# Weighing V in fp16 pairs inside clustered attention

## The chip, the cores and the metric

One core of one Trainium2 chip runs the whole program. The metric is device time in microseconds, of the slowest core where there are several; here there is one.

## What is computed

Clustered attention, followed by two layers of experts (top-1 routing of 1536 tokens). Only attention is touched by the change:

```python
scores = scale * np.matmul(q, k.transpose(0, 1, 3, 2))      # q, k, v: 2 x 8 x 768 x 64, fp32
scores = np.where(q_assign == k_assign, scores, -1e9)       # cluster = argmax over 16 centroids
attn = np.exp(scores - scores.max(-1))
attn = attn / (attn.sum(-1) + 1e-9)
out = np.matmul(attn, v)
```

A query none of whose keys is in its cluster gets the mean of V. The result is fp32.

## The kernel before

The program has a raw program for each engine, with semaphores between them; nothing is moved by a scheduler, so every engine does its work in the order in which it is written. `attention` goes over 16 heads (2 batches of 8) one after the other. `steps` (L163) calls `step(s, par)` for s = -1, 0, 1, then a rolled loop for heads 2 to 13, then 14 and 15. Step s holds three heads at once: the scores and the weighing of head s, the cluster masks and the row maxima of head s + 1, and the turning and cluster logits of head s + 2. `has(s, n)` says whether head s + n exists. `par` chooses one of two buffers.

A head has 768 keys in T = 6 tiles of 128 (`kt`), and 768 queries in two halves of 384 (`HALF`).

- TensorE, `step` (L516): `scores` (L481) makes the transposed scores of a tile of keys in two parts, an exact fp32r part with hi and lo of q and k (`QA`, `KA`) and one with `QB`, `KB`, whose rows hold the hi halves, the masks and the negated row maxima in three parts. `weigh` (L496) multiplies the exps of one key tile (`probs`, fp32, weights of 128 columns) with V and a column of ones (`v1`, 65 columns) and adds into the PSUM tile `pv`, three products for each half. Between these, `other` pops work of the next heads from the list `between`: `turn_b` (L455, transposed masks), twelve products of `maxima` (L463, u = 0 to 11, which alternate between the PSUM tiles `turn0` and `turn1`), four `turn_a` (L431), `turn_m` (L473, transposed maxima). How many go where is the table `BETWEEN` (L154). At the end of a step stands `assign` (L441), the cluster logits.
- ScalarE: the exps of a tile (L245, two of 384), behind tile 1 the masks into `QB` (L250), behind tile 2 `hi` (L225 and L226), at the end the two copies of `QA` (L232) and the maxima into `QB` (L258).
- VectorE: masks into `KB` (L376), twelve reductions of the maxima (L382), seven small operations that each wait for the one before (L388 to L395), two copies of `KA` (L349), the denominators and the output of the head (L403 to L410), the masks of head s + 2 (L356 to L364), the sum of V (L343).
- GpSimd: `lo` (L273 and L274: q and k less their hi halves), `double_hi` (L282 and L285: copies to other partitions), the sum of two output parts (L306), the copy of V into `v1` (L293).
- SyncE: q, k and v of head s + 2 (L199), behind the last head the first experts' weights (L1133) and the copies of x.

An exp may start when its buffer of `probs` (two) is free and the scores are there; `scores` of tile kt waits for the exps of tile kt - 2; `weigh` waits for the exps of its half. `turn_m` waits for the seven small operations, `assign` for the copies of `QA` and `KA`.

## Time and profile before

| | us |
|---|---|
| runs, median of 3 (lowest to highest) | 748.81 (747.76 to 752.83) |
| the profiled execution | 747.8 |
| its span | 746.1 |

| engine | busy us | share of the span | instructions |
|---|---|---|---|
| TensorE, products (PE) | 724.5 | 97% | 5200 |
| TensorE, weight loads (PEld) | 643.3 | 86% | 5209 |
| VectorE (DVE) | 443.8 | 59% | 917 |
| ScalarE (ACT) | 247.2 | 33% | 441 |
| GpSimd (POOL) | 172.1 | 23% | 229 |

The span is counted from the first instruction to the last; the profiled execution is 1.7 us longer than it. Weight loads overlap products, and products overlap each other, so the time between two starts on TensorE, not the duration of one, tells what a product costs. Attention ends at about 326 us, and the rest are the two layers of experts. A row of a timeline gives start, length, engine, line, operation, `out<-in` and, in square brackets, how long the engine was idle before it and what it waited for.

### The profile page before, as it was taken

The numbers are of one execution on the slowest core, as the hardware profiler recorded it, in microseconds if no ns is written. First come the engines' busy times: TensorE is split into PE (matmuls) and PEld (weight loads), VectorE is DVE, ScalarE is ACT, GpSimd is POOL, SyncE is SP. The second block draws the span as 40 slices with busy tenths as digits, with TensorE's granted clock in tenths as the row PEclk, the third lists the DMA queues.
The fourth block names the chain that finished last, engine by engine and source line by source line (L and its number), as shares of the span: only waits on it lengthen the run. The fifth ranks groups of instructions, "written<-read, shape, count | busy, mean of one in ns | idle before, by whom it ended". The sixth has DMA issues, their size and how long they took to land.

```text
span 746.1 us, 15191 instructions
## 1 busy us (share of the span) xinstructions
PE 724.5 (97%) x5200; PEld 643.3 (86%) x5209; DVE 443.8 (59%) x917; ACT 247.2 (33%) x441; POOL 172.1 (23%) x229
## 2 busy tenths in 40 slices
PE   8999999999999999997999999988999999999996
PEld 4799999999999999974898989945799998999995
DVE  5788888888888888546644655527533442624521
ACT  2344444444444444442214351313221232321300
POOL 4222222222222222001221312200222221312211
PEclk9999999999999999999999999999999999999998
DMA  3001110111011197041656998455445646662100
GB/s 99 18 18 33 32 33 31 32 32 32 32 32 32 32 341 309 1 165 34 232 185 233 365 325 313 145 203 204 143 156 167 231 170 233 256 231 92 40 28 29
DMA packets 43598, 99.16 MB, mean 133 GB/s; under 512 B 5139, under 2 KB 11283, under 8 KB 43568
## 3 DMA queue, kind: packets, MB, share of 16 engines
q1 hardware_dynamic: 36096, 84.45, 31.8%
q0 software_dynamic: 4544, 12.70, 5.4%
q10 hardware_dynamic: 2928, 1.62, 0.7%
q8 instruction: 17, 0.28, 0.2%
q14 instruction: 13, 0.11, 0.0%
HBM read 87.64 MB, written 13.11 MB: 135 GB/s over the span
## 4 chain that ended last, share of the span: by engine, by line
PE 49%; DVE 3%; DMA 2%; issue 1%; ACT 0%; POOL 0%; POOLq 0%; ACTq 0%; DVEq 0%
PE hT_ps_layer L1009 25%; PE y_ps_layer L1022 6%; PE y_ps_layer L1026 6%; PE y_ps_layer L1029 6%; PE x_turn_layer L996 2%; DMA x<-x_mid 1%; PE hT_ps_layer L951 1%; PE hT_ps_layer L938 1%; PE hT_ps_layer L936 1%; PE x_turn_layer L926 1%; DVE row_one_hot_layer L838 0%; DMA x_tile_layer<-x_src,token_to_read_layer 0%; DMA x_mid<-y_out_layer,y_token_layer 0%; PE count_ps_layer L926 0%; PE rank_ps_layer L926 0%
## 5 line engine op out<-in xcount | busy, mean ns | idle before, releaser
L1009 PEld LDWEIGHTS hT_ps_layer<-xT_layer,w 128*128 128x128 f32 x1664 | 189.6, 192 | 3.4 <-DVE xT_layer L871 1.4
L1009 PE MATMUL hT_ps_layer<-xT_layer,w 128*128 128x128 f32 x1664 | 190.2, 276 | 0.5 <-issue 0.5
L505 PE MATMUL pv<-v_and_one,probs 128*128 128x65 f32 x1152 | 147.9, 270 | 0.0
L505 PEld LDWEIGHTS pv<-v_and_one,probs 128*128 128x128 f32 x1152 | 146.8, 192 | 0.6
L382 DVE TENSOR_REDUCE max_halves<-turn 128x1 f32<-128x384 f32 x192 | 102.4, 555 | 39.3 <-PE turn L470 35.6
L245 ACT ACTIVATE probs<-scores 128x384 f32<-128x384 f32 x192 | 82.0, 492 | 85.2 <-PE scores L491 84.8
L760 ACT ACTIVATE hT_hi_layer<-hT_ps_layer 128x512 fp32r<-128x512 f32 x52 | 31.1, 597 | 238.9 <-PE hT_ps_layer L1009 238.9
L898 DVE SCALAR_TENSOR_TENSOR hT_lo_layer<-hT_ps_layer,hT_hi_layer 128x512 fp32r<-128x512 f32 x52 | 34.7, 689 | 88.0 <-ACT hT_hi_layer L760 75.5
L878 DVE TENSOR_TENSOR w_lo<-w,w_hi 128x1024 fp32r<-128x1024 f32 x64 | 74.0, 1220 | 0.0
L755 ACT ACTIVATE w_hi<-w 128x1024 fp32r<-128x1024 f32 x64 | 62.4, 1047 | 27.0 <-issue 27.0
L470 PE MATMUL turn<-kB,qB 96*128 96x384 f32 x192 | 69.8, 402 | 0.0
L1022 PE MATMUL y_ps_layer<-w_hi,hT_hi_layer 128*128 128x512 f32 x208 | 58.6, 404 | 0.0
L1029 PE MATMUL y_ps_layer<-w_hi,hT_lo_layer 128*128 128x512 f32 x208 | 56.6, 394 | 0.0
L1026 PE MATMUL y_ps_layer<-w_lo,hT_hi_layer 128*128 128x512 f32 x208 | 56.5, 394 | 0.0
L1073 POOL DMA_INDIRECT out_dram<-y_out_layer,y_token_layer x16 | 19.8, 1239 | 148.1 <-DVE y_out_layer L909 148.1
L909 DVE TENSOR_SCALAR y_out_layer<-y_ps_layer,slot_gate_layer 128x512 f32<-128x512 f32 x16 | 12.0, 751 | 64.1 <-PE y_ps_layer L1029 64.1
L491 PE MATMUL scores<-qA,kA 128*128 128x384 f32 x192 | 49.7, 353 | 0.0
L491 PE MATMUL scores<-qB,kB 99*128 99x384 f32 x192 | 47.0, 340 | 0.0
L1026 PEld LDWEIGHTS y_ps_layer<-w_lo,hT_hi_layer 128*128 128x128 f32 x208 | 39.1, 188 | 9.0
L1029 PEld LDWEIGHTS y_ps_layer<-w_hi,hT_lo_layer 128*128 128x128 f32 x208 | 38.9, 188 | 9.1 <-DVE hT_lo_layer L898 0.5
L1022 PEld LDWEIGHTS y_ps_layer<-w_hi,hT_hi_layer 128*128 128x128 f32 x208 | 37.2, 189 | 6.7
L282 POOL CAST qB<-qA 64x768 fp32r<-64x768 f32 x16 | 13.1, 817 | 125.4 <-DVE kA L349 125.4
(194 smaller groups left out, 864.7 us busy)
## 6 DMA issues: line engine op xcount, KB each, us to landing
w<-in_moe_w_dram SPq DMA_DIRECT2D x32, 2048.0 KB, 9.6
qkv_raw<-in_q_dram SPq DMA_DIRECT2D x16, 192.0 KB, 2.4
qkv_raw<-in_k_dram SPq DMA_DIRECT2D x16, 192.0 KB, 2.5
qkv_raw<-in_v_dram SPq DMA_DIRECT2D x16, 192.0 KB, 3.2
x_src<-x SPq DMA_DIRECT2D x2, 1536.0 KB, 11.9
x_mid<-x SPq DMA_DIRECT2D x2, 1536.0 KB, 14.7
...
```

The lines of the kernel that those rows point to most:

```text
L245: nc.scalar.activation(probs[kt % 2][:, n * HALF:(n + 1) * HALF], sc[kt % 2][:, n, 0:HALF], ACT.Exp, scale=SCALE).then_inc(probs_ready, 1)
L382: nc.vector.tensor_reduce(mh[:, u // 2, u % 2:u % 2 + 1], turn[b][:, 0:HALF], AX.X, ALU.max).then_inc(turn_free[b], 1)
L470: nc.tensor.matmul(turn[b][:, 0:HALF], QB[par][0:ROWS_MASK, t * P:(t + 1) * P], KB[par][0:ROWS_MASK, n * HALF:(n + 1) * HALF], start=True, ...
L491: m = nc.tensor.matmul(sc[kt % 2][:, n, 0:HALF], lhs[:, kt * P:(kt + 1) * P], rhs[:, n * HALF:(n + 1) * HALF], start=(part == 0), stop=(pa ...
L505: m = nc.tensor.matmul(pv_o[:, t, :], probs[kt % 2][:, t * P:(t + 1) * P], v1[par][:, kt, :], start=False, stop=(kt == T - 1), skip_group_ ...
L755: nc.scalar.activation(W2H[par][:, c, :], W2[par][:, c, :], ACT.Copy).then_inc(w2_hi, 1)
L878: nc.vector.tensor_tensor(W2L[:, c, :], W2[par][:, c, :], W2H[par][:, c, :].bitcast(F32), ALU.subtract).then_inc(w2_lo, 1)
L898: nc.vector.scalar_tensor_tensor(out=hL[:, half, :].rearrange("p c n -> p (c n)"), in0=hp[n][:], scalar=0.0, in1=hH[:, half, :].rearrange( ...
L1009: t = nc.tensor.matmul(hp[n][:, i * P:(i + 1) * P], W1[par][:, c, f * P:(f + 1) * P], xT[:, c, :], start=(c == 0), stop=(c == CD - 1))
L1022: nc.tensor.matmul(yp[:], hH[:, f, :], W2H[par][:, f, :], start=(f == 0), stop=False)
L1026: nc.tensor.matmul(yp[:], hH[:, f, :], W2L[:, f, :], start=False, stop=False)
L1029: t = nc.tensor.matmul(yp[:], hL[:, f, :], W2H[par][:, f, :], start=False, stop=(f == CF - 1))
```

## The change

The exps of a tile are made twice from the same scores, once in fp32 (`probs`) and once in fp16 (`p_hi`). The rest `probs - p_hi` is taken in fp16 (`p_lo`) by GpSimd for tiles 0 to 4 and by VectorE for tile 5. V is scaled by a power of two and split into `v_hi` (ScalarE) and `v_lo` (VectorE), both fp16. In place of one fp32 product stand three of 16 bit: `p_hi` with `v_hi`, `p_hi` with `v_lo`, `p_lo` with `v_hi`. The first two of a half are `weigh_hi`, the third is `weigh_lo`, which stands one tile later. `probs`, `p_hi` and `p_lo` have three buffers. The sum of V is made on TensorE by twelve products with ones (`sum_v`), not by VectorE.

All of V is loaded at the start by ScalarE's queue in four quarters into the memory of the experts' W1 (`v_all`). VectorE takes the largest absolute value of each quarter (`v_topmost`), then of all (`v_power`, with one transposition on TensorE, `turn_v`), and makes from its exponent bits the factors `v_up` and `v_down`. The exponents are raised by 7 with the maxima (`SHIFT`).

Moved: the copies of `KA` from VectorE to ScalarE (`evac_a`, now four); `double_hi` from GpSimd to two DMAs of SyncE; the factor of the masks from VectorE to ScalarE's copy; the load of the first two W1 behind the last `v_lo`; GpSimd's sum of a head's output into the next step; `BETWEEN` has five places for each tile.

```diff
-    BETWEEN = ((0, 0, 1), (0, 1, 1), (1, 2, 1), (1, 2, 1), (2, 2, 0), (2, 1, 0))
+    BETWEEN = ((0, 0, 0, 0, 0), (0, 0, 0, 1, 0), (0, 0, 0, 1, 1), (1, 0, 1, 1, 1), (1, 1, 1, 1, 0), (1, 1, 1, 0, 0))
...
+            def double_hi(i, par):
+
+                b, m = use_a(i, 3)
+                sp.wait_ge(turn_free[b], m + 1)
+                sp.dma_start(QB[par][0:D, :].bitcast(F32), QA[par][0:D, :].bitcast(F32)).then_inc(hi_doubled, 16)
+                sp.dma_start(KB[par][0:D, :].bitcast(F32), KA[par][D:2 * D, :].bitcast(F32)).then_inc(hi_doubled, 16)
...
+            def split_v(i, par):
+                act.wait_ge(v_scaled, 1)
+                wait(act, pv_done, T * (i - 1))
+                nc.scalar.activation(v_hi[par][:, :, 0:D], v_of(i), ACT.Copy, scale=v_up).then_inc(v_hi_done, 1)
...
                         for n in range(2):
+                            half = slice(n * HALF, (n + 1) * HALF)
                             act.wait_ge(scored[kt % 2], T * s + 2 * (kt // 2) + n + 1)
-                            nc.scalar.activation(probs[kt % 2][:, n * HALF:(n + 1) * HALF], sc[kt % 2][:, n, 0:HALF],
-                                                 ACT.Exp, scale=SCALE).then_inc(probs_ready, 1)
+                            nc.scalar.activation(probs[slot][:, half], sc[kt % 2][:, n, 0:HALF], ACT.Exp, scale=SCALE).then_inc(probs_ready, 1)
+                            nc.scalar.activation(p_hi[slot][:, half], sc[kt % 2][:, n, 0:HALF], ACT.Exp, scale=SCALE).then_inc(probs_ready, 1)
...
+                    if kt == 3 and has(s, 1) and not first:
+                        split_v(s + 1, 1 - par)
...
+                if first:
+                    split_v(0, 0)
             run(act, step)
...
+            def rest(i, kt):
+
+                slot = kt % RING_P
+                wait(pool, pv_done, T * i + kt - RING_P + 1)
+                for n in range(2):
+                    half = slice(n * HALF, (n + 1) * HALF)
+                    pool.wait_ge(probs_ready, 4 * (T * i + kt) + 2 * n + 2)
+                    nc.gpsimd.tensor_tensor(p_lo[slot][:, half], probs[slot][:, half], p_hi[slot][:, half], ALU.subtract).then_inc(p_lo_pool, 1)
...
+                if c:
+                    rest(s, 0)
+                    rest(s, 1)
+                if c and not (isinstance(s, int) and s == 0):
+                    add_up(s - 1)
+                if c:
+                    rest(s, 2)
+                if a:
+                    lo_q(s + 2, par)
+                if c:
+                    rest(s, 3)
+                if a:
+                    lo_k(s + 2, par)
+                if c:
+                    rest(s, 4)
...
-                link(nc.vector.tensor_tensor(eq[:], lg[:], top[:, 1, :].unsqueeze(2).to_broadcast([P, 2 * T, C]), ALU.is_equal))
-                if par is not None:
-                    nc.vector.tensor_scalar(maskb[par][:, :, 0:C], eq[:, 0:T, :], MASKED, None, ALU.mult).then_inc(mask_steps, 1)
-                    nc.vector.tensor_scalar(maskb[par][:, :, 2 * C:3 * C], eq[:, T:2 * T, :], -1.0, 1.0, ALU.mult, ALU.add).then_inc(mask_steps, 1)
...
+                best = lambda n: top[:, 1, n:n + T].unsqueeze(2).to_broadcast([P, T, C])
+                nc.vector.tensor_tensor(maskb[par][:, :, 0:C], lg[:, 0:T, :], best(0), ALU.is_equal).then_inc(mask_steps, 1)
+                nc.vector.tensor_tensor(maskb[par][:, :, 2 * C:3 * C], lg[:, T:2 * T, :], best(T), ALU.not_equal).then_inc(mask_steps, 1)
...
+                        if u == 5 and first:
+                            v_topmost(2)
+                        if u == 9 and not first:
+                            split_v(i, 1 - par)
...
+                if first:
+                    v_topmost(3)
+                    v_power()
+                    split_v(0, 0)
                 if has(s, 0):
+                    kt = T - 1
+                    slot = kt % RING_P
+                    dve.wait_ge(pv_done, T * s + kt - RING_P + 1)
+                    for n in range(2):
+                        half = slice(n * HALF, (n + 1) * HALF)
+                        dve.wait_ge(probs_ready, 4 * (T * s + kt) + 2 * n + 2)
+                        nc.vector.tensor_tensor(p_lo[slot][:, half], probs[slot][:, half], p_hi[slot][:, half], ALU.subtract).then_inc(p_lo_dve, 1)
                     dve.wait_ge(pv_done, T * s + T)
...
+            def weigh_hi(i, par, kt, half):
+                pe.wait_ge(probs_ready, 4 * (T * i + kt) + 2 * half + 2)
                 for t in range(half * T // 2, (half + 1) * T // 2):
-                    m = nc.tensor.matmul(pv_o[:, t, :], probs[kt % 2][:, t * P:(t + 1) * P], v1[par][:, kt, :],
+                    p = p_hi[kt % RING_P][:, t * P:(t + 1) * P]
+                    nc.tensor.matmul(pv_o[:, t, :], p, v_hi[par][:, kt, 0:D + 1], start=False, stop=False, skip_group_check=True)
+                    m = nc.tensor.matmul(pv_o[:, t, 0:D], p, v_lo[par][:, kt, :], start=False, stop=False, skip_group_check=True)
...
+            def weigh_lo(i, par, kt, half):
+                if kt == T - 1:
+                    pe.wait_ge(p_lo_dve, 2 * i + half + 1)
+                else:
+                    pe.wait_ge(p_lo_pool, POOL_P * i + 2 * kt + half + 1)
+                for t in range(half * T // 2, (half + 1) * T // 2):
+                    m = nc.tensor.matmul(pv_o[:, t, :], p_lo[kt % RING_P][:, t * P:(t + 1) * P], v_hi[par][:, kt, 0:D + 1],
                                          start=False, stop=(kt == T - 1), skip_group_check=True)
...
                 for kt in range(T):
...
+                    for half in range(2):
+                        if c and kt > 0:
+                            weigh_lo(s, par, kt - 1, half)
+                        other(BETWEEN[kt][2 * half])
+                        if c:
+                            weigh_hi(s, par, kt, half)
+                        if half == 0:
+                            other(BETWEEN[kt][1])
+                    other(BETWEEN[kt][3])
                     if c and kt + 2 < T:
                         scores(s, par, kt + 2, last)
-                    other(BETWEEN[kt][2])
+                    other(BETWEEN[kt][4])
                 other(len(between))
+                if c:
+                    for half in range(2):
+                        weigh_lo(s, par, T - 1, half)
                 if a:
                     assign(s + 2, par)
+                if first:
+                    turn_v()
```

How this moves instructions is shown at three places. The line numbers of the rows after the change are those of the changed kernel.

ScalarE, the exps of tiles 1 and 2 of a head (`probs` and `probs_hi`) with the masks' copy `qB` between them. Before:

```order
L245 ACTIVATE probs<-scores 128x384 x4
L250 ACTIVATE qB<-turn 32x768
L245 ACTIVATE probs<-scores 128x384 x2
L225 ACTIVATE q_features<-qkv_raw 128x6x64
L226 ACTIVATE k_features<-qkv_raw 128x6x64
```

ScalarE at the same place after the change; the first four rows are tile 1, tile 0 has four more like them ahead:

```order
L304 ACTIVATE probs<-scores 128x384
L305 ACTIVATE probs_hi<-scores 128x384
L304 ACTIVATE probs<-scores 128x384
L305 ACTIVATE probs_hi<-scores 128x384
L309 ACTIVATE qB<-turn 32x768
L304 ACTIVATE probs<-scores 128x384
L305 ACTIVATE probs_hi<-scores 128x384
L304 ACTIVATE probs<-scores 128x384
L305 ACTIVATE probs_hi<-scores 128x384
L273 ACTIVATE q_features<-qk_raw 128x6x64
```

Ahead of the masks' copy stand eight exps where four stood, and ahead of the copy of q twelve where six stood.

TensorE around the first products of the maxima (`turn<-kB,qB`), from the transposed masks on. Before:

```order
L460 MATMUL turn<-ident_b,masks 96x128 x6
L505 MATMUL pv<-v_and_one,probs 128x65 x6
L470 MATMUL turn<-kB,qB 128x384
L491 MATMUL scores<-qA,kA 128x384 x2
L491 MATMUL scores<-qB,kB 128x384 x2
```

TensorE there after the change, up to the first product of the maxima; the last rows before it are `weigh_hi` of tile 2:

```order
L555 MATMUL turn<-ident_b,masks 96x128 x6
L586 MATMUL scores<-qA,kA 128x384 x2
L586 MATMUL scores<-qB,kB 128x384 x2
L615 MATMUL pv<-v_hi_and_one,probs_lo 128x65 x3
...
L605 MATMUL pv<-v_lo,probs_hi 128x64
L565 MATMUL turn<-kB,qB 128x384
L586 MATMUL scores<-qA,kA 128x384 x2
```

The first product of the maxima moved from behind the products of tile 1 to behind those of tile 2.

VectorE at the end of a head, from the small operations of the maxima to the denominator. Before:

```order
L394 CAST max_parts<-max_rest 128x6
L395 TENSOR_TENSOR max_parts<-max_rest,max_parts 128x6
L349 CAST kA<-turn 128x384 x2
L403 SCALAR_TENSOR_TENSOR denominator<-pv,no_key 128x6
L405 RECIPROCAL denominator<-denominator 128x6
```

VectorE there after the change:

```order
L481 CAST max_parts<-max_rest 128x6
L482 TENSOR_TENSOR max_parts<-max_rest,max_parts 128x6
L494 TENSOR_TENSOR probs_lo<-probs,probs_hi 128x384 x2
L498 SCALAR_TENSOR_TENSOR denominator<-pv,no_key 128x6
L500 RECIPROCAL denominator<-denominator 128x6
```

In the place of two copies that TensorE's `assign` waits for stand two subtractions that its last `weigh_lo` of the head waits for.

## Rows read from the trace of the kernel before

**Rows 1.** The page, part 1: busy us, share of the span, instructions.
```profile
PE 724.5 (97%) x5200; PEld 643.3 (86%) x5209; DVE 443.8 (59%) x917; ACT 247.2 (33%) x441; POOL 172.1 (23%) x229
```

**Rows 2.** Timeline of TensorE in one step: start us, us, engine, line, operation, tiles.
```profile
150.40 0.78 PE L505 MATMUL pv<-v_and_one,probs 128*128 128x65 f32 x6
150.98 0.42 PE L470 MATMUL turn<-kB,qB 96*128 96x384 f32 x1
...
161.04 0.84 PE L451 MATMUL cluster_logits_ps<-centroids_T,qA 128*128 x6
...
162.40 0.94 PE L491 MATMUL scores<-qA,kA 128*128 128x384 f32 x4
...
166.35 0.53 PE L460 MATMUL turn<-ident_b,masks 128*96 128x128 bf16 x6
166.72 1.50 PE L505 MATMUL pv<-v_and_one,probs 128*128 128x65 f32 x12
...
181.11 0.94 PE L491 MATMUL scores<-qA,kA 128*128 128x384 f32 x4
```

**Rows 3.** Timeline of TensorE in the routing of the first experts.
```profile
351.44 0.56 PE L986 MATMUL rank_ps_layer<-tile_gate_parts_layer,row_one_hot_layer 128*128 128x72 bf16 x12 [0.86 <-DVE tile_gate_parts_layer L859]
351.84 1.46 PE L951 MATMUL hT_ps_layer<-blank 128*128 128x512 bf16 x6
```

**Rows 4.** Timeline of ScalarE in the same step as rows 2.
```profile
148.96 0.87 ACT L245 ACTIVATE probs<-scores 128x384 f32<-128x384 f32 x2
149.72 0.53 ACT L225 ACTIVATE q_features<-qkv_raw 128x384 fp32r<-128x384 f32 x1
...
163.55 1.64 ACT L245 ACTIVATE probs<-scores 128x384 f32<-128x384 f32 x4 [1.67 <-PE scores L491]
166.92 0.80 ACT L250 ACTIVATE qB<-turn 32x768 fp32r<-32x768 bf16 x1 [1.73 <-PE turn L460]
```

**Rows 5.** Timeline of VectorE in the same step.
```profile
151.44 0.56 DVE L382 TENSOR_REDUCE max_halves<-turn 128x1 f32<-128x384 f32 x1 [0.29 <-PE turn L470]
152.29 1.69 DVE L382 TENSOR_REDUCE max_halves<-turn 128x1 f32<-128x384 f32 x3 [0.29 <-PE turn L470]
...
158.24 0.17 DVE L388 TENSOR_REDUCE max_negated<-max_halves 128x6 f32<-128x12 f32 x1
...
159.79 1.02 DVE L349 CAST kA<-turn 128x384 fp32r<-128x384 f32 x2
160.73 0.15 DVE L403 SCALAR_TENSOR_TENSOR denominator<-pv,no_key 128x6 f32<-128x6 f32 x1
...
163.96 0.54 DVE L358 TENSOR_TENSOR cluster_best<-cluster_logits,cluster_top 128x192 f32<-128x192 f32 x1
...
166.14 0.81 DVE L343 TENSOR_REDUCE v_sum<-qkv_raw 128x64 f32<-128x384 f32 x1
```

**Rows 6.** Timeline of GpSimd in the same step.
```profile
163.26 1.03 POOL L306 TENSOR_TENSOR x<-o_attn,o_mean 128x384 f32 x1 [0.48 <-DVE o_mean L410]
164.23 0.64 POOL L293 COPY v_and_one<-qkv_raw 128x384 f32<-128x384 f32 x1
```

**Rows 7.** Durations of two lines of VectorE: ns min/median/max, first and last start.
```profile
L358 DVE TENSOR_TENSOR cluster_best<-cluster_logits,cluster_top x16: 357/542/549, 14.5 to 295.2; 128x192 f32<-128x192 f32 x16
...
L406 DVE TENSOR_SCALAR denominator<-no_key x16: 171/670/686, 48.6 to 323.7; 128x6 f32<-128x6 f32 x16
```

**Rows 8.** Timeline before the first head: VectorE, then ScalarE.
```profile
27.43 0.17 DVE L395 TENSOR_TENSOR max_parts<-max_rest,max_parts 128x6 bf16<-128x6 f32 x1
...
30.82 1.28 ACT L245 ACT_TABLE_LOAD   x1
32.42 1.64 ACT L245 ACTIVATE probs<-scores 128x384 f32<-128x384 f32 x4 [0.32 <-PE scores L491]
```

**Rows 9.** The page, part 6: DMA issues, count, KB each, us to landing.
```profile
w<-in_moe_w_dram SPq DMA_DIRECT2D x32, 2048.0 KB, 9.6
qkv_raw<-in_q_dram SPq DMA_DIRECT2D x16, 192.0 KB, 2.4
```

234 lines of the change are left out of this document (137 added, 97 removed).

## The prediction

> **What bounds the kernel now.** First the page's busy times, then the timeline of one step of one head engine by engine, then the durations by line. The page says that TensorE is busy 97% of the span [rows 1]. TensorE's timeline shows why: a step begins with `scores` at 162.40 and the next one at 181.11, so a step is 18.7 us, and inside it no matmul row carries an idle time [rows 2]. The other engines wait for TensorE: ScalarE's rows before an exp or before `L250` end in `<-PE scores`, `<-PE turn` [rows 4], VectorE's reductions have 0.29 us of `<-PE turn` ahead of it [rows 5], and of GpSimd's operations, six a step, [rows 6] show the last two. So the step is TensorE's sum, and 15 such steps (heads 0 to 14) stand between the start and the last head. Behind attention nothing is changed except when the first experts' weights come.
>
> **TensorE's part.** Three fp32 products of one half take 150.98 - 150.40 = 0.58 us [rows 2]; a step has 12 halves, 7.0 us, which go. In their place stand 108 products with 16 bit operands and 12 for `sum_v`, 120 in all, each with a 128 column weight load. The trace has no 65 column fp16 product. The nearest row is twelve bf16 products of 72 columns with 128 column weights, all inputs ready: the next line starts 351.84 - 351.44 = 0.40 us later, 0.033 each [rows 3]. The other end is `L460`, six with 96 column weights and 128 moving columns in 166.72 - 166.35 = 0.37, 0.062 each [rows 2]. I take 0.033: 120 x 0.033 = 4.0 us, and TensorE's sum falls to 18.7 - 7.0 + 4.0 = 15.7 us. With 0.062 it is 19.1.
> The Trainium skill, "TensorE: Matmul & The Clock Gate", section "Back-to-back issue gap", speaks against this: it gives about 81 ns per product for a stream of weight load and product at 128 columns. By that page 120 products would be 9.7 us and TensorE's sum 21.4. The row at 72 columns measures 33 ns, so the row decides.
>
> **What takes TensorE's place.** TensorE's sum would allow 15.7 us, but the step is a ring of waits, and the change lengthens the other engines' part of it. I walk it, t = 0 at the start of `scores`.
> 1. The first exp starts at 163.55 - 162.40 = 1.15 [rows 2, 4]. Exps follow each other in 0.38 us (two in 149.72 - 148.96 = 0.76) [rows 4]. Each tile is now exponentiated twice, so tiles 0 and 1 are eight exps, not four: the last starts at 1.15 + 7 x 0.38 = 3.8 and is done at 4.3 (0.49 for one).
> 2. `turn_b` stands behind `weigh_hi(1, half 1)` on TensorE, which needs that last exp: six products, 0.2 us, so it starts at 4.6. `L250` starts 166.92 - 166.35 = 0.57 after `turn_b` [rows 2, 4], at 5.2, and takes 0.80. The exps of tile 2 are queued behind it on ScalarE: 6.0 to 6.0 + 3 x 0.38 + 0.49 = 7.6.
> 3. The first of the 12 maxima products stands behind `weigh_hi(2, half 1)`, which needs them: t = 7.9. Before, it stood right behind the products of tile 1, ahead of everything that waits for tile 2.
> 4. VectorE's reduction starts 151.44 - 150.98 = 0.46 after its product [rows 2, 5], at 8.4. Three in a row take 1.69, so 0.565 each [rows 5], twelve 6.8 us. `split_v` stands behind the tenth, two gaps, 0.5 together, come from the `scores` that stand between maxima products: 8.4 + 6.8 + 0.55 + 0.5 = 16.2.
> 5. The seven small operations take 159.79 - 158.24 = 1.55 [rows 5]: t = 17.8. `turn_m` waits for them, as before.
> 6. New: VectorE then subtracts the rests of tile 5, two operations, and `weigh_lo(5)` waits for them. Their form is not in the trace; 192 elements of this kind take 0.357 [rows 7], a reduction of 384 takes 0.56 [rows 5]. I take 0.55 each: 18.9. The two `kA` copies that stood here (1.02) [rows 5] are gone, but those were hidden under TensorE's products; what replaces them is waited for.
> 7. `weigh_lo(5)` takes 0.1, and `assign` behind it 162.40 - 161.04 = 1.36 [rows 2]. The next `scores` start at 18.9 + 0.1 + 1.36 = 20.4.
> So the step is 20.4 us instead of 18.7: plus 1.7, times 15 = 25.5 us.
>
> **What is hidden.** ScalarE's sum per step is 24 exps x 0.38 = 9.1, six copies of 384 at no more than 0.53 = 3.2 [rows 4], `L250` and `L258` 1.6, `split_v` 0.5: 14.4 of 20.4. The tail of a head on VectorE, from `L403` to the masks' end, is 166.14 - 160.73 = 5.4 [rows 5], less one operation of the form of `L358` (0.357 alone [rows 7]) that goes. It starts 0.2 behind `weigh_lo(5)`, at t = -1.1, and ends at 4.0, when `turn_b` at 4.6 has not yet come: hidden by 0.6 us, and lost one for one behind that. `v_sum` (0.81) goes, it was hidden. The doubling of q and k by SyncE's DMA instead of GpSimd starts at t = 18.5 and is needed at 7.9 of the next step, 9.8 us later, and 192 KB land in 2.4 [rows 9]; queued behind it on SyncE are only the loads of the next q and k. W1 now waits for the last `v_lo`, in the step before the last: it is needed behind the routing, so I count nothing.
> GpSimd gets ten subtractions per step. Two operations of 384 elements start 164.23 - 163.26 = 0.97 apart [rows 6]; bounds 0.6 (the copy lasts 0.64) and 1.03. With 0.97 its order is ten rests, two of q and k, one sum: the first at t = 2.1, the twelfth (tile 4, half 0) done at 2.1 + 12 x 0.97 = 13.7, and with what VectorE takes from it 14.5. TensorE needs it for the eleventh maxima product at about 14.7: just in time. At 1.03 it is 15.3, and 0.3 us on the step.
>
> **Start and end.** Before the first head VectorE takes the top of V in four reductions of 1536 elements, each 0.56 + 1152 elements at the pace of 384 in 0.4, 1.75 us. Two of them lie in waits. The third stands in the maxima, the fourth behind the small operations, whose last one ends at 27.6 [rows 8]: 27.6 + 3.5 = 31.1. Then 2 small operations, a transposition, a reduction and 8 small operations, 0.2 each with 0.7 for the passes over TensorE: 34.0. ScalarE's `split_v` stands ahead of the exps and of their table load: 34.0 + 0.5 + 1.28 = 35.8 for the first exp, 32.42 before [rows 8]. That is 3.4 us. A quarter of V is 768 KB, and 2048 KB land in 9.6 [rows 9], so V's load beside the first q and k adds between 0 and 3.6; I take 0.5, since q's and k's own 192 KB are issued at the same time. The last head has no other work to mix in: 24 exps and 11 GpSimd operations end at about its old length, I take plus 0.5.
> Sum: 25.5 + 3.9 + 0.5 = 29.9 us. The profiled execution took 747.8 us (span 746.1); 747.8 + 29.9 = 777.7. The median of the runs is 1.0 above it, 748.8: so 779 us.
>
> **The rivals.**
> A, faster: the ring has more slack than I see, and the step follows TensorE. TensorE's 15.7 and the wait at the step's end, from its last transposition to the rests of tile 5, about 1.5: 17.2 us. 15 x (17.2 - 18.7) = -22.5, and 4.4 for start and end: 748.8 - 18 = 731 us. For it speaks that the trace's rings have waits everywhere on the other engines (VectorE is busy 59%). Against it: steps 1 to 3 above have no free choice, they are queue orders. It decides if the first maxima product comes before t = 6. Chance 0.11.
> B, the same ring a little shorter, the rest of the step 18.5 to 19.2: within 1%. Chance 0.07.
> C, slower still: GpSimd and VectorE get in each other's way. `L406`, six elements, takes 171 ns at the least and 670 in the median; `L358` 357 and 542 [rows 7]; the `L358` of 0.54 at 163.96 [rows 5] lies on GpSimd's two operations from 163.26 to 164.87 [rows 6]. Now GpSimd works 13 x 0.97 = 12.6 us of a step, not some 5, and beside it stand on VectorE four mask operations, `split_v` and, if GpSimd is late, the small operations. If each of the two sides waits for the other, GpSimd's twelfth operation is done at 15.4, the eleventh maximum starts 0.7 later, and three small operations wait 0.1 to 0.5 each: 21.4 us. 15 x 2.7 + 4.4 = 45: 793 us. Chance 0.13.
> The Trainium skill, "SBUF — State Buffer", section "Who interferes with whom", says that a VectorE instruction with two inputs in SBUF, or in a two-port mode, and a GpSimd instruction that reads SBUF block each other for the whole instruction. The 670 against 171 ns agree. It is the mechanism of C.
> D, the change doesn't do what it says: three 16 bit products cost TensorE as much as one of fp32, because each has its own weight load. At 0.062 us each (`L460`) TensorE's sum is 19.1, above the old 18.7, and the seven groups of products that stand on the ring grow by 0.5: a step of 20.9, 15 x 2.2 + 4.4 = 37, 786 us. Against it stands [rows 3]. Chance 0.05. By the 81 ns of the page named above the sum alone would be 21.4, which would make it some 794 us.
>
> **How the numbers follow.** The forecast 0.64, A 0.11, B 0.07, C 0.13, D 0.05. The forecast's own range: maxima product 0.5 earlier or later, rests 0.36 to 0.9, GpSimd 0.6 to 1.03, the start 0 to 8: 19.6 to 21.0 us a step, 764 to 790 us. To leave out no more than 2 in 10 the range reaches down to 756, towards B (741 to 756 stay outside), and up over C's own 793 to 796. A measurement of this kernel tells about 1% from no change. Faster by over 1%: A, 0.11. Within 1%: 0.07. Slower: 0.82.
>
> **What would show it.** In the profile after: the distance between two starts of `scores` at a head's begin (20.4); the first `L470` product of a step near t = 7.9, with TensorE idle before it on ScalarE's exps; `weigh_lo(5)` waiting for VectorE's rests; twelve fp16 products in 0.4 us; the first exp at 35.8. Wrong if TensorE is still without idle time in a step (A or D), or if GpSimd's rests end TensorE's waits at tile 2 to 4 (C).

## The result, and the profile after

| | kernel before | kernel after |
|---|---|---|
| median of the runs | 749.09 us (747.76 to 752.83) | 779.77 us (777.82 to 782.19) |
| ratio, 95% interval | | 1.040 (1.036 to 1.045) |
| profiled execution: own time, span | 747.8, 746.1 us | 782.2, 780.5 us |
| mean granted clock of TensorE over the span | 0.992 (1.00 in every step of attention) | 0.973 |

The kernel is 4.0% slower. Medians are over all runs and ratios over the undisturbed ones: of the experiments below, those of 814.5 and 754.4 us have one run in a slower state in their median. The profiled execution was 2.4 us above the median, so what follows adds up to 34.4 us and not to 30.7. First the page's busy times of after, which answer to [rows 1]:

```profile
PE 713.3 (91%) x5937; PEld 587.2 (75%) x5946; DVE 447.1 (57%) x916; ACT 342.0 (44%) x681; POOL 277.7 (36%) x341
```

TensorE's busy time fell by only 11 us. That is not the work taken out: a row's length reaches past the start of the next one, so short gaps count as busy, and a step at a lower clock counts longer. What changed is that TensorE is no longer busy throughout, 91% where it was 97%. The timeline of TensorE in one step of after (columns as in [rows 2]):

```profile
162.65 0.96 PE L586 MATMUL scores<-qA,kA 128*128 128x384 f32 x4
...
167.24 0.53 PE L555 MATMUL turn<-ident_b,masks 128*96 128x128 bf16 x6
...
169.56 0.20 PE L604 MATMUL pv<-v_hi_and_one,probs_hi 128*128 128x65 f16 x1 [0.92 <-ACT probs_hi L305]
...
170.33 0.20 PE L604 MATMUL pv<-v_hi_and_one,probs_hi 128*128 128x65 f16 x1 [0.32 <-ACT probs_hi L305]
170.37 0.20 PE L605 MATMUL pv<-v_lo,probs_hi 128*128 128x64 f16 x1
...
170.63 0.41 PE L565 MATMUL turn<-kB,qB 96*128 96x384 f32 x1
...
181.03 0.50 PE L615 MATMUL pv<-v_hi_and_one,probs_lo 128*128 128x65 f16 x6
181.55 0.84 PE L546 MATMUL cluster_logits_ps<-centroids_T,qA 128*128 x6
...
182.91 0.96 PE L586 MATMUL scores<-qA,kA 128*128 128x384 f32 x4
```

The step is 182.91 - 162.65 = 20.26 us. A 16 bit product starts 0.04 after its neighbour (170.33, 170.37). Before the first maxima product `L565` TensorE now waits for ScalarE's second exps, which [rows 2] did not show. ScalarE and VectorE in the same step:

```profile
163.82 0.49 ACT L304 ACTIVATE probs<-scores 128x384 f32<-128x384 f32 x1 [2.13 <-PE scores L586]
...
166.43 0.56 ACT L305 ACTIVATE probs_hi<-scores 128x384 f16<-128x384 f32 x1
167.81 0.80 ACT L309 ACTIVATE qB<-turn 32x768 fp32r<-32x768 bf16 x1 [0.82 <-PE turn L555]
168.64 0.49 ACT L304 ACTIVATE probs<-scores 128x384 f32<-128x384 f32 x1
...
178.83 1.03 ACT L280 ACTIVATE qA<-turn 128x384 fp32r<-128x384 f32 x2 [2.67 <-PE turn L533]
```

```profile
165.73 0.97 DVE L446 TENSOR_TENSOR masks<-cluster_logits,cluster_top 128x96 bf16<-128x96 f32 x1
...
171.08 0.56 DVE L465 TENSOR_REDUCE max_halves<-turn 128x1 f32<-128x384 f32 x1 [2.32 <-PE turn L565]
...
177.58 1.01 DVE L465 TENSOR_REDUCE max_halves<-turn 128x1 f32<-128x384 f32 x2
178.71 0.17 DVE L475 TENSOR_REDUCE max_negated<-max_halves 128x6 f32<-128x12 f32 x1
...
180.18 1.03 DVE L494 TENSOR_TENSOR probs_lo<-probs,probs_hi 128x384 f16<-128x384 f32 x2
```

Before, VectorE waited 0.56 us for the first maxima product of a step (the row below is from the step at 162.40) and 0.29 for later ones [rows 5]; now it waits 2.32 for the first.

```profile
168.49 0.56 DVE L382 TENSOR_REDUCE max_halves<-turn 128x1 f32<-128x384 f32 x1 [0.56 <-PE turn L470]
```

GpSimd in the step of after:

```profile
164.77 3.59 POOL L349 TENSOR_TENSOR probs_lo<-probs,probs_hi 128x384 f16<-128x384 f32 x4 [8.14 <-ACT probs_hi L305]
...
175.01 1.79 POOL L349 TENSOR_TENSOR probs_lo<-probs,probs_hi 128x384 f16<-128x384 f32 x2
```

Where the 34.4 us of the two profiled executions come from: the first exp starts 6.84 us later (39.26 against 32.42 [rows 8]); from there to the first operation behind head 14 (`L498`, before `L403`) it is 306.1 us against 277.1, plus 29.0; the last head takes 13.55 against 13.71; the rest 421.6 against 422.9. Most steps are 20.2 us, plus 1.5 each. Five are longer. The busy table by step, two ordinary ones and two of the five (the last three columns: granted clock, DMA share, GB/s):

```profile
141.14:161.31 20.17, 17.63 (x193) 13.83 (x193) 14.86 (x36) 14.24 (x34) 11.75 (x13) 1.00 0.14 39
161.31:181.57 20.26, 17.70 (x193) 13.86 (x193) 14.86 (x36) 14.28 (x34) 11.76 (x13) 1.00 0.13 39
181.57:202.62 21.05, 18.68 (x193) 14.97 (x193) 14.86 (x35) 14.10 (x34) 11.75 (x13) 0.92 0.13 37
98.63:120.89 22.26, 20.20 (x193) 16.46 (x193) 13.98 (x36) 14.00 (x34) 11.72 (x13) 0.85 0.13 37
```

VectorE, ScalarE and GpSimd are not busy longer in the two long steps; TensorE's clock is lower there and its busy time longer. The timeline shows where it falls, here at the end of the third:

```profile
198.45 0.82 PE L533 MATMUL turn<-ident,q_features 128*128 128x128 f32 x3 [0.54 <-DVE max_halves L465]
199.41 0.88 PE L533 MATMUL turn<-ident,q_features 128*128 128x128 f32 x3
200.09 1.69 PE L533 MATMUL turn<-ident,k_features 128*128 128x128 f32 x6
```

Behind a wait for the last maxima the six transpositions of k take 1.69 us, where they take 1.09 at full clock. One such wait does not decide it: the next step has the same one and keeps its clock.

```profile
219.50 0.52 PE L533 MATMUL turn<-ident,q_features 128*128 128x128 f32 x3 [0.54 <-DVE max_halves L465]
```

The five longer steps hold 5.3 us over the ordinary ones, and only four of them, with 4.5 us, are at a lower clock. The fifth (77.61 to 98.63, 21.02 us) has the granted clock at 1.00. There a VectorE operation of the masks that takes 0.36 alone stands beside GpSimd's rests, and TensorE waits for the masks:

```profile
80.86 1.11 DVE L442 TENSOR_TENSOR cluster_logits<-cluster_best,tie 128x192 f32<-128x192 f32 x1
```
```profile
83.90 0.53 PE L555 MATMUL turn<-ident_b,masks 128*96 128x128 bf16 x6 [0.41 <-DVE masks L446]
```

That is rival C's mechanism on the ring, in one step of fifteen.

### The profile page after: what moved, and what is told of

It is laid out like the page before. It is cut to its first block, busy times and chain, and to the rows that moved or that the text cites. A ratio compares the mean times of both kernels' runs of the same rounds, so it can differ in the third digit from the quotient of the medians.

```text
span 780.5 us, 17315 instructions
## 1 busy us (share of the span) xinstructions
PE 713.3 (91%) x5937; PEld 587.2 (75%) x5946; DVE 447.1 (57%) x916; ACT 342.0 (44%) x681; POOL 277.7 (36%) x341
## 3 DMA queue, kind: packets, MB, share of 16 engines
q10 hardware_dynamic: 5040, 4.77, 1.9%
## 4 chain that ended last, share of the span: by engine, by line
PE 47%; DVE 2%; DMA 2%; issue 1%; ACT 0%; POOL 0%; POOLq 0%; ACTq 0%; DVEq 0%
PE hT_ps_layer L1132 24%; PE y_ps_layer L1145 6%; PE y_ps_layer L1149 6%; PE y_ps_layer L1152 6%; PE x_turn_layer L1119 2%; DMA x<-x_mid 1%; PE hT_ps_layer L1074 1%; PE hT_ps_layer L1061 1%; PE hT_ps_layer L1059 1%; PE x_turn_layer L1049 1%; DVE row_one_hot_layer L961 0%; DMA x_tile_layer<-x_src,token_to_read_layer 0%; DMA x_mid<-y_out_layer,y_token_layer 0%; PE count_ps_layer L1049 0%; PE rank_ps_layer L1049 0%
## 5 line engine op out<-in xcount | busy, mean ns | idle before, releaser
L349 POOL TENSOR_TENSOR probs_lo<-probs,probs_hi 128x384 f16<-128x384 f32 x160 | 143.6, 922 | 151.6 <-ACT probs_hi L305 151.6
L465 DVE TENSOR_REDUCE max_halves<-turn 128x1 f32<-128x384 f32 x192 | 99.6, 553 | 48.0 <-PE turn L565 44.4
L304 ACT ACTIVATE probs<-scores 128x384 f32<-128x384 f32 x192 | 102.8, 535 | 33.0 <-PE scores L586 32.6
L305 ACT ACTIVATE probs_hi<-scores 128x384 f16<-128x384 f32 x192 | 104.5, 545 | 0.0
L604 PE MATMUL pv<-v_hi_and_one,probs_hi 128*128 128x65 f16 x576 | 63.0, 198 | 26.2 <-ACT probs_hi L305 25.3
L565 PE MATMUL turn<-kB,qB 96*128 96x384 f32 x192 | 79.1, 422 | 3.0 <-DVE max_halves L465 1.5
L604 PEld LDWEIGHTS pv<-v_hi_and_one,probs_hi 128*128 128x128 f16 x576 | 41.7, 99 | 42.0 <-ACT probs_hi L305 33.0
L1196 POOL DMA_INDIRECT out_dram<-y_out_layer,y_token_layer x16 | 19.7, 1233 | 147.1 <-DVE y_out_layer L1032 147.1
L605 PE MATMUL pv<-v_lo,probs_hi 128*128 128x64 f16 x576 | 61.6, 196 | 0.0
L586 PE MATMUL scores<-qA,kA 128*128 128x384 f32 x192 | 52.9, 372 | 0.0
L615 PE MATMUL pv<-v_hi_and_one,probs_lo 128*128 128x65 f16 x576 | 49.6, 197 | 2.8 <-POOL probs_lo L349 2.4
```

The source lines that it names most:

```text
L304: nc.scalar.activation(probs[slot][:, half], sc[kt % 2][:, n, 0:HALF], ACT.Exp, scale=SCALE).then_inc(probs_ready, 1)
L305: nc.scalar.activation(p_hi[slot][:, half], sc[kt % 2][:, n, 0:HALF], ACT.Exp, scale=SCALE).then_inc(probs_ready, 1)
L349: nc.gpsimd.tensor_tensor(p_lo[slot][:, half], probs[slot][:, half], p_hi[slot][:, half], ALU.subtract).then_inc(p_lo_pool, 1)
L465: nc.vector.tensor_reduce(mh[:, u // 2, u % 2:u % 2 + 1], turn[b][:, 0:HALF], AX.X, ALU.max).then_inc(turn_free[b], 1)
L565: nc.tensor.matmul(turn[b][:, 0:HALF], QB[par][0:ROWS_MASK, t * P:(t + 1) * P], KB[par][0:ROWS_MASK, n * HALF:(n + 1) * HALF], start=True, ...
L586: m = nc.tensor.matmul(sc[kt % 2][:, n, 0:HALF], lhs[:, kt * P:(kt + 1) * P], rhs[:, n * HALF:(n + 1) * HALF], start=(part == 0), stop=(pa ...
```

## The experiments

t is counted from the start of `scores` of a step. Ratios are to the kernel before, run beside each.

**Maxima products earlier.**
```diff
-BETWEEN = (..., (0, 0, 0, 1, 0), (0, 0, 0, 1, 1), (1, 0, 1, 1, 1), (1, 1, 1, 1, 0), (1, 1, 1, 0, 0))
+BETWEEN = (..., (0, 0, 0, 1, 2), (0, 0, 1, 1, 1), (1, 0, 1, 1, 1), (1, 1, 1, 0, 0), (1, 0, 0, 0, 0))
```


> The kernel after, with three maxima products placed ahead of the products of tile 2 that wait for ScalarE (two right behind scores(3), one between the halves of tile 2). Theory, the ring of waits: the first reduction moves from t = 8.43 to about 6.45 (L309 of the masks ends at 5.96, then product and 0.46), and everything behind it by the same 2.0 us: a step of 18.3 instead of 20.26, 15 x -1.95 = -29, so about 751 us. Rival C, GpSimd's ten rests set the step: it does not start its rests earlier, so 20.2 us a step and 780 us. Rival TensorE-bound: no change either, 780.

Measured: 757.4 us, ratio 1.014 (1.012 to 1.015), a step of 18.93 for the ordinary ones. That is 22 us by the medians, 20 by the ratios (1.040 to 1.014), of the change's 31, by the place of three products alone. The step is 0.6 us longer than expected, and the time 6 us. The rows of a step whose `scores` start at 152.71:

```profile
159.06 0.59 PE L565 MATMUL turn<-kB,qB 96*128 96x384 f32 x2 [0.47 <-DVE kB L459]
```
```profile
157.86 0.95 DVE L459 CAST kB<-turn 32x768 fp32r<-32x768 bf16 x1 [1.12 <-PE turn L555]
159.51 2.11 DVE L465 TENSOR_REDUCE max_halves<-turn 128x1 f32<-128x384 f32 x4 [0.69 <-PE turn L565]
...
165.30 1.09 DVE L431 SCALAR_TENSOR_TENSOR v_lo<-w,v_scale_bits,v_hi_and_one 128x384 f16<-128x384 f16 x1
```

The first reduction comes at 6.80, not 6.45: TensorE waits for VectorE's kB copy (0.95), which I had left out beside ScalarE's 0.80. And `split_v` takes 1.09 where it took 0.61: GpSimd's last two rests run from 165.05 to 167.16 here, beside it. The ring decides, and behind it contention is at work.

**The rests of tile 5 on GpSimd.**
```diff
+                    rest(s, 5)
...
-                        nc.vector.tensor_tensor(p_lo[slot][:, half], probs[slot][:, half], p_hi[slot][:, half], ALU.subtract)...
```


> The kernel after, with the rests of tile 5 on GpSimd instead of VectorE. Theory: VectorE's 1.03 us leave the ring, but ScalarE's four copies L280 end at t = 18.33 and assign waits for them, so the gain is cut to about 0.5 us: a step of 19.7, about 772 us. Rival C, GpSimd sets the step: two operations of 0.9 more on it make a step 1.8 longer, 22.0, about 806 us; in the weaker form, GpSimd and VectorE block each other on SBUF, the seven small operations behind the maxima (0.17 each, 1.43 together) now lie beside GpSimd's rests and grow to 0.5 each, and the step stays at 20.2 or above, 780 us or more.

Measured: 814.5 us, ratio 1.085 (1.080 to 1.089). The expectation of my theory was wrong by 42 us. The time is above the rival's 806 too. The rival's weaker form had the blocking, but on the seven small operations, which take 0.17 to 0.18 here; it falls on `split_v`. `split_v` over 14 steps (ns min/median/max), then TensorE and GpSimd in one of the steps of 24.5 us, and VectorE's row between them:

```profile
L429 DVE SCALAR_TENSOR_TENSOR v_lo<-w,v_scale_bits,v_hi_and_one x14: 606/1908/2062, 76.7 to 373.9; 128x384 f16<-128x384 f16 x12, 128x384 f16<-128x384 f32 x2
```
```profile
290.38 1.63 PE L577 MATMUL scores<-qA,kA 128*128 128x384 f32 x4
...
308.44 0.52 PE L524 MATMUL turn<-ident,q_features 128*128 128x128 f32 x3 [1.91 <-DVE max_halves L463]
...
309.74 1.69 PE L524 MATMUL turn<-ident,k_features 128*128 128x128 f32 x6
```
```profile
303.89 3.52 POOL L346 TENSOR_TENSOR probs_lo<-probs,probs_hi 128x384 f16<-128x384 f32 x4
```
```profile
305.85 1.98 DVE L429 SCALAR_TENSOR_TENSOR v_lo<-w,v_scale_bits,v_hi_and_one 128x384 f16<-128x384 f16 x1
```

GpSimd works on four rests without a pause from 303.89 to 307.41. VectorE's `split_v` starts within them and ends at 307.83, behind the last. TensorE waits 1.91 us for the maxima behind it, and then its clock falls: the six transpositions of k take 1.69 us and not 1.09. The step had also begun at the lower clock: its first four `scores` products, at 290.38, take 1.63 us and not 0.94. The one step with the clock at 1.00 throughout took 20.34 us, and in it `split_v` took 1.15; the others took 21.2 to 24.8 at clocks of 0.77 to 0.94. So the blocking (1.4 us in the step shown) and the lower clock together cost up to 4.5 us of a step.

**Both edits together.**

> Both edits together (maxima early, all rests on GpSimd). Theory: the last reduction ends at t = 14.0, the copies L280 at 16.5, assign right behind: a step of 17.9, 15 x -2.4 = -36, about 744 us, 4 to 5 us below the kernel before. If the two edits gave only the larger of their gains: 751. Rival C: as in the run with the rests alone, 780 or more, since GpSimd's twelve rests and three others are 13.5 us plus its waits and the last rest now starts behind all of them.

Measured: 770.4 us, ratio 1.031 (1.028 to 1.035), steps of 19.6. It lies between the theory's 744 to 751 and the rival's 780. GpSimd's rests start beside the masks, and the same blocking shows in other places:

```profile
158.32 1.12 DVE L440 TENSOR_TENSOR cluster_logits<-cluster_best,tie 128x192 f32<-128x192 f32 x1
...
172.18 0.84 DVE L475 TENSOR_SCALAR max_negated<-max_negated 128x6 f32<-128x6 f32 x1
```

Alone these take 0.36 and 0.17. `split_v` stands beside four rests here too, but takes 1.09 and not 1.98:

```profile
169.38 1.09 DVE L429 SCALAR_TENSOR_TENSOR v_lo<-w,v_scale_bits,v_hi_and_one 128x384 f16<-128x384 f16 x1
```
```profile
169.13 3.86 POOL L346 TENSOR_TENSOR probs_lo<-probs,probs_hi 128x384 f16<-128x384 f32 x4
```

The four rests take 3.86 where they took 3.52 in the run before: here VectorE waited for one of them and then GpSimd for VectorE, while there VectorE, starting in the third, waited for the third and the fourth. What decides between the two is open. The edits are not additive: moving the rests of tile 5 to GpSimd loses 13 us of the 20 that the earlier maxima win.

**One exp instead of two.**
```diff
-                            nc.scalar.activation(probs[slot][:, half], sc[kt % 2][:, n, 0:HALF], ACT.Exp, scale=SCALE)...
```


> The kernel after with ScalarE's twelve fp32 exps of a step left out: the fp32 probabilities are a constant 1.0, so the rests are 1 minus the high half; every rest, product and wait stays. Theory: tiles 0 and 1 are exponentiated by t = 2.8 instead of 4.34, but VectorE's masks end at 4.05 and set turn_b at 4.1 instead of 4.59; the copy L309 ends at 5.5, tile 2 has two exps and not four (6.4 instead of 7.62), and the first reduction starts at about 7.0 instead of 8.43: a step of 18.8, 15 x -1.4 = -21, about 759 us. Rival C, GpSimd's rests or their contention set the step: 20.2, 780 us.

Measured: 837.1 us, but this total can't be used: with other outputs of attention the experts got other tokens, and the page counts 1984 products of `hT` where after has 1664. Attention itself, to the same operation behind the last head, took 345.99 us against 358.90 in after. That is 12.9 less, not 21; the steps are 19.6 to 20.1, not 18.8. What cut the gain, in a step whose `scores` start at 156.43:

```profile
161.20 0.53 PE L558 MATMUL turn<-ident_b,masks 128*96 128x128 bf16 x6 [0.63 <-DVE masks L448]
```
```profile
158.31 0.98 DVE L444 TENSOR_TENSOR cluster_logits<-cluster_best,tie 128x192 f32<-128x192 f32 x1
...
160.10 0.96 DVE L448 TENSOR_TENSOR masks<-cluster_logits,cluster_top 128x96 bf16<-128x96 f32 x1
```

TensorE now waits for the masks, at t = 4.77: with the exps gone from there GpSimd starts its rests earlier (t = 1.73, where it was 2.12), and one more of VectorE's mask operations is blocked. My walk had the masks done at 4.05; they end at 4.63.

**Products of zeros in TensorE's waits.**
```diff
+            def keep_up(n):
+                for _ in range(n):
+                    nc.tensor.matmul(pv[:, 456:512], blank[:, 0:P], blank[:, 0:56], start=False, stop=False, ...)
```


> The kernel after, with products of zeros (56 columns, bf16, about 0.03 us each) in three of TensorE's waits in a step: 10 ahead of the high products of tile 1 (wait 0.41), 26 ahead of those of tile 2 (wait 0.92), 12 ahead of the first transposition of q behind the maxima (wait 0.54). They do nothing for the output. Theory that the idle gaps let TensorE's clock fall: the granted clock stays at full speed in all steps, the five steps of 21.0 to 22.3 become 20.2, and the time falls by 5 to 6 us, to about 774. Rival, the clock falls whatever TensorE does in these waits: 780 and again a mean clock of 0.97 to 0.98. If the products reach past the waits, up to 0.3 us a step, 4 us, come on top in either case.

Measured: 779.7 us, ratio 1.043 (1.042 to 1.044): no gain, by its number the rival's 780. In the profiled execution two steps are long (22.5 and 21.1) where after had five, but the rest took up to 20.35 and the mean clock was 0.975. It neither proves nor refutes the cause. The two runs with fp16 below do that for the kernel before; that the falls in after have the same cause is argued from them, not shown.

**TensorE's relief alone.**
```diff
-    v1 = [sb(f"v_and_one{i}", [P, T, D + 1], F32) for i in range(2)]
-    probs = [sb(f"probs{i}", [P, S], F32) for i in range(2)]
+    v1 = [sb(f"v_and_one{i}", [P, T, D + 2], F16) for i in range(2)]
+    probs = [sb(f"probs{i}", [P, S], F16) for i in range(2)]
```


> The kernel before, with probabilities, values and ones in fp16 and one product each: the rests are left out, and so is everything the change added to ScalarE, GpSimd and VectorE; the order is that of before. It shows what TensorE's relief alone is worth. Theory: TensorE's sum is 18.7 - 7.0 + 36 x 0.033 = 12.9, so the ring of the other engines decides: exps of tiles 0 and 1 done at 2.8, VectorE's masks at 3.8, turn_b, L250 from 4.4 to 5.2, the first reduction at 5.7 and the last end at 13.0, small operations 14.6, copies of k 15.7, assign 17.0. A step of 17.0, 15 x -1.7 = -26, about 722 us. Rival D, 16 bit products cost TensorE as much as the fp32 one (or 0.062 each): 18.7 a step or at most 1 us less, 733 to 747. If VectorE's and TensorE's order had the slack of rival A: 15 us a step, 693.

Measured: 754.4 us, ratio 1.008 (1.005 to 1.011). With 5.8 us of TensorE's work taken out of every step and nothing added the kernel is slightly slower than before, and 32 us above the expected 722. Two of its steps, busy times by engine:

```profile
89.00:106.64 17.64, 14.57 (x114) 11.29 (x112) 15.13 (x37) 8.42 (x18) 5.21 (x6) 1.00 0.11 34
124.50:145.70 21.20, 19.30 (x114) 15.41 (x112) 15.67 (x37) 8.42 (x18) 5.20 (x6) 0.69 0.09 28
```

At full clock a step is 17.7 us, and TensorE's waits in it are all for VectorE: 0.83 us for the masks, 0.92 for the `KB` copy, 0.42 for the `KA` copies, and three shorter ones for the reductions. So the ring through VectorE (15.1 us busy) stood 1.1 us behind TensorE's sum in the kernel before, and no relief of TensorE could bring more than that a step in this order. At the lower clock a step is 21.2.

**The same with products of zeros in its waits.**

> The kernel before with one fp16 product (rests left out, as in the run of that name), and with products of zeros (56 columns, bf16, about 0.03 us each) where TensorE waited there: 20 ahead of turn_b (wait 0.81), 26 ahead of the first maxima product (0.92), 14 ahead of the last products of a head (0.54 of wait behind them). Theory, TensorE's clock falls because of these gaps, and steps of 21.3 us come from nothing else: every step takes the 17.7 to 17.9 us of the undisturbed ones, and the time is 747 - 14 x 1.0 - 4.4 (last head) - 1.9 (first) = about 727 us. Rival, the gaps are not the cause: again some steps of 21, 750 or more.

Measured: 724.8 us, ratio 0.968 (0.965 to 0.972), mean clock 0.995. Thirteen steps take 17.4 to 17.9, the last one ahead of the last head 16.6:

```profile
134.06:151.83 17.77, 16.16 (x174) 12.93 (x172) 15.13 (x37) 8.43 (x18) 5.23 (x6) 1.00 0.10 33
```

60 products that compute nothing, in each step, take 30 us off the kernel, as expected (727). Nothing else differs between the two programs, so the idle time of TensorE is the cause of the lower clock here. The Trainium skill, "TensorE: Matmul & The Clock Gate", section "Part 1: The HAM clock gate", describes a gate that sets the clock by how busy TensorE has been; the pair of runs agrees with it (754.4 and 724.8 us).

**The scale as a constant.**
```diff
+            for at, value in ((v_up, 4096.0), (v_down, 1 / 4096), (v_scale[:, 3:4], 1 / 4096 / S)):
+                nc.vector.memset(at, value).then_inc(v_topped, 1)
...
-                    v_topmost(3)
-                    v_power()
```


> The kernel after, with the power of two as constants (4096 and 1/4096) written at the start: the four reductions over all values, the ten small operations and the transposition behind them are left out, V's four loads and everything in the steps stay. Theory: the start was 6.8 us later than before (39.26 against 32.42 for the first exp), of which 5.5 to 6 are this search and its lower TensorE clock; so the first exp comes at about 33.5 and the time falls by 5.5 us, to 774. Rival, V's load (3 MB beside q and k) holds the start: it gains under 2 us, 778 or more.

Measured: 775.2 us, ratio 1.038 (1.036 to 1.040), 4.6 below after by the medians and only 2 by the ratios (1.040 to 1.038), whose intervals overlap. Its first exp starts at 31.36, where 33.5 was expected: the search costs 7.9 us at the start, more than its whole lateness of 6.8, and with V's load still in place the first exp is no later than before. The gain in the medians is smaller than that; the two profiled executions stand on opposite sides of their medians (782.2 and 772.6), so the 7.9 is a reading of one execution each.

**All rests on GpSimd, V split in front.**
```diff
                     dve.sem_inc(turn_free[b], 1)
+                    if not first:
+                        split_v(i, 1 - par)
                     for u in range(2 * T):
-                        if u == 9 and not first:
-                            split_v(i, 1 - par)
```


> All rests on GpSimd, as in the run that took 814 us, with one edit more: V is split at the step's begin, on ScalarE ahead of the first exp and on VectorE behind the kB copy, where VectorE waits 2.3 us for the first maxima product. Theory, that run lost its time because split_v on VectorE stood beside GpSimd's back-to-back rests, took 1.9 us in place of 0.6, left TensorE idle for 2 us, and TensorE's clock then fell: here the two reductions behind it come 1.9 us earlier, no gap of 2 us remains, the rests of tile 5 and split_v are off the ring, a step is 19.1 to 19.7, about 765 us. Rival, GpSimd's thirteen to fifteen operations themselves are too many: 800 or more.

Measured: 766.3 us, ratio 1.025 (1.021 to 1.028), steps of 19.4, mean clock 0.995 in the profiled execution and 0.987 in the others, as expected (765). ScalarE's part of the split moved to the step's begin as well. From 814 to 766 by the place of these two operations, of which VectorE's of 0.6 us is the one that had been blocked:

```profile
L429 DVE SCALAR_TENSOR_TENSOR v_lo<-w,v_scale_bits,v_hi_and_one x14: 620/830/958, 62.5 to 315.1; 128x384 f16<-128x384 f16 x12, 128x384 f16<-128x384 f32 x2
```

GpSimd's load is the same as in the run of 814. So what cost the 48 us was not how much GpSimd does, but which of VectorE's operations stands beside it.

**A mixture: two tiles whole, four in pairs.** Tiles 0 and 1 keep the fp32 product, with V scaled in fp32 too; the maxima stand early; V is split at the step's begin.
```diff
+                if kt < WHOLE:
+                    pe.wait_ge(probs_ready, exps(i, kt) + half + 1)
+                    for t in range(half * T // 2, (half + 1) * T // 2):
+                        m = nc.tensor.matmul(pv_o[:, t, :], probs[kt % RING_P][:, t * P:(t + 1) * P], v_whole[par][:, kt, :], ...)
```


> A mixture: tiles 0 and 1 of the keys are weighed with the single fp32 product as before (V scaled by the same power), tiles 2 to 5 in fp16 pairs; the maxima products stand early as in the run with that edit; both parts of splitting V stand in front, in waits of ScalarE and VectorE in which GpSimd does nothing. Theory of the ring: TensorE's sum is 15.7 + 4 x 0.25 = 16.7; exps of tiles 0 and 1 end at 2.8, masks at 3.4 since GpSimd is silent beside them, L309 from 4.0 to 4.8, first reduction 5.6, last end 12.8, small operations 14.3, rests of tile 5 15.4, the copies L280 15.6, assign, next scores at 17.2. 15 x (17.2 - 18.7) = -22.5, and +6 at the start: about 731 us, 2% below the kernel before. Rival TensorE-bound or 16 bit products too dear: 745 to 757. Rival C, GpSimd decides: its nine operations are 8.5 us from t = 5.6, its last rest at 14.1 plus what VectorE takes, so about 731 to 740 as well; only the rows would tell.

Measured: 781.4 us, ratio 1.046 (1.044 to 1.048), 50 us above the expectation; a step is 19.7 to 21.0 and not 17.2. In a step that starts at 182.10:

```profile
187.36 0.50 PE L567 MATMUL turn<-ident_b,masks 128*96 128x128 bf16 x6
...
197.03 0.27 PE L635 MATMUL pv<-v_hi_and_one,probs_lo 128*128 128x65 f16 x3 [0.86 <-POOL probs_lo L363]
```

I had counted TensorE's sum but not its order at the step's begin: `turn_b` stands behind two tiles of fp32 products and comes at 5.26, and at the end TensorE waits for GpSimd's last rest.

**The mixture in another order.**
```diff
-BETWEEN = ((0, 0, 0, 0, 0), (0, 0, 0, 1, 2), (0, 0, 1, 1, 1), (1, 0, 1, 1, 1), (1, 1, 1, 0, 0), (1, 0, 0, 0, 0))
+BETWEEN = ((0, 0, 0, 0, 1), (0, 0, 0, 2, 1), (0, 1, 0, 1, 1), (1, 0, 1, 1, 1), (1, 1, 0, 0, 1), (0, 0, 0, 0, 0))
```


> The mixture again (tiles 0 and 1 with the fp32 product), with turn_b ahead of the products of tile 1, two maxima products ahead of scores(3), the first transposition of q ahead of the rests of tile 4, and GpSimd's sum of the last head behind the masks instead of among the rests. In the first mixture turn_b came at t = 5.26 because both tiles' fp32 products and scores(2) stood ahead of it. Theory: turn_b at 4.0, L324 from 4.5 to 5.3, first reduction 6.1 (7.45 in the first mixture), last end 13.2, small operations 14.8, rests of tile 5 15.9, next scores 17.4 to 17.8: 15 x -1.1 + 6 = about 737 us. Rival, GpSimd's rests of tile 4 or VectorE blocked beside GpSimd end the step: 19 to 20 us a step as in the first mixture, 755 to 775.

GpSimd's sum of a head's output also stands behind the masks now.

Measured: 744.7 us, ratio 0.997 (0.994 to 0.999), steps of 17.6 and two of 19.2. The same arithmetic as the run of 781, and 8 us above the expected 737: the first head took 20.5 us from its first exp where before took 15.8, and the two longer steps hold 3.1. In a step that starts at 150.20 `turn_b` comes at 3.99. VectorE's masks are not blocked and end at 3.09, as in the run of 781, where `turn_b` had to stand behind TensorE's own products until 5.26:

```profile
154.19 0.50 PE L569 MATMUL turn<-ident_b,masks 128*96 128x128 bf16 x6
```
```profile
153.04 0.25 DVE L460 TENSOR_TENSOR masks<-cluster_logits,cluster_top 128x96 bf16<-128x96 f32 x1
```

**That one with products of zeros, and the table load early.**
```diff
+            nc.scalar.activation(v_top[:, 7:8], cen_s[:, 0:1], ACT.Exp, scale=0.0)
...
+                between += [lambda n=n: (keep_up(8 if c and n in (0, 3) else 0), turn_a(s + 2, par, n)) ...
+                between += [lambda: (keep_up(8 if c else 0), turn_m(s + 1, 1 - par, not a))] if b else []
```


> The second mixture (744.7 us, steps of 17.6 and two of 19.2) with eight products of zeros each ahead of the first and the fourth transposition of q and k and ahead of turn_m, where TensorE waits, and with one exp of a single column behind the square root at the start, so that ScalarE's table load lies in its wait there. Theory: the two steps of 19.2, in which the granted clock had fallen, become 17.6 (3 us), and the table load of 1.28 leaves the path to the first exp: 744.7 - 3.2 - 1.3 = about 740 us, 1% below the kernel before. Rival, the falls have nothing to do with the waits, or the products of zeros reach past them (0.3 us a step): 743 to 748.

Measured: 739.5 us, ratio 0.987 (0.985 to 0.990), as expected (740): the fastest version that keeps pairs, in four of six tiles, 1.3% below the kernel before and 5% below after. Its profiled execution was its slowest (744.1), so the split of the gain is not clean: steps are 17.7 to 17.9 with one of 18.3, at a clock of 1.00, in which `split_v` took 1.46, and the first exp is at 39.01, no earlier than in the run before it, because the search for the power took longer in this execution.

## Why the prediction was right

The ring was read right in its ordinary step, 20.26 us where 20.4 was forecast. That the time met to 1 us (779 and 779.8) is luck: the sum for the profiled execution was 777.7, and that took 782.2; only the medians agree, because the forecast took the median to lie 1.0 above the profiled execution and in after it lies 2.4 below. By its steps:

1. First exp at 1.15, eight exps done at 4.3: 1.17 and 4.34.
2. `turn_b` at 4.6, the copy at 5.2, tile 2's exps 6.0 to 7.6: 4.59, 5.16, 5.99 to 7.62.
3. First maxima product at 7.9: 7.98. The first experiment confirms that this step is the main cause: placed earlier, it gives back 20 to 22 of the 31 us.
4. Reductions from 8.4 to 16.2: 8.43 to 15.94.
5. Small operations done at 17.8: 17.48.
6. Rests of tile 5, taken as 0.55 each: 0.52 each, done at 18.56.
7. Next `scores` at 20.4: 20.26.

TensorE's part: 0.033 a product was right (0.03 to 0.04), which refutes rival D. The whole sum of 15.7 no run isolates; TensorE's busy time in a step of after is 17.7, with short gaps in it. Rival A fell with step 3.

What was wrong:
- "15 x 1.7 = 25.5". It was 29.0. An ordinary step costs 1.5, 22.5 in all. The falls of the clock in four steps, which no step and no rival had, add 4.5, and the blocked masks of one step 0.8. The rest, 1.2, lies in heads 0 and 14, which lost 2.65 and 2.35, less what rounding takes off. [Rows 2] could not show the falls, since TensorE had no idle time there.
- The start, 3.9: it was 6.84, and the search is 7.9 by the constant's run. The small operations ended 3.0 us later than in the kernel before (30.59 and 27.60), where 1.75 was counted for the third reduction: TensorE's twelve products of head 0's cluster logits took 1.43 and 1.44 at the lower clock where before took 0.81 and 0.82. And "0.7 for the passes over TensorE" was 2.68 of waiting, because the transposition of the tops stands on TensorE's queue behind the transpositions of q and k (the six of q took 1.49 us, also at the lower clock), `turn_m` and `assign`:

```profile
35.44 0.29 DVE L418 TENSOR_REDUCE v_top<-pv 128x1 f32<-128x128 f32 x1 [2.68 <-PE pv L622]
```

- The last head, plus 0.5: minus 0.16. Behind attention, 0: minus 1.3, for which I have no cause.
- GpSimd's 0.97 an operation: 0.89 to 0.92 for a rest. It works 11.75 us a step.
- Rival C had 0.13 and "793". Its blocking is there in after, in the masks (0.97 us where 0.25 is the time without GpSimd beside it), but in all steps but one lies in the 0.6 us that step 2 leaves. What I had sized wrong is its reach: in the run of 814 us it adds 1.4 us to one operation, and the lower clock behind it comes on top. The change missed this by little: `split_v` starts at 177.06, GpSimd's last rest ends at 176.80. Two more rests a step cost 35 us.
- Slips of the arithmetic: B's steps of 18.5 to 19.2 are 750 to 761 us by its own sum, so only those up to 18.9 are within 1%; C's sum gives 794 and not 793; the bounds of the forecast's own range, taken together, give 763 to 792 and not 764 to 790. None of them touches the outcome.

The fp16 runs also say what a relief of TensorE could have brought: 5.8 us a step, of which the change's three products take out about 3, were worth at most 1.1, because VectorE's ring came next, and only with the clock held.
